# Gaps between the SBUF tiles that TensorE reads, so that they start at many different distances modulo 512 bytes

## The reference, cut to what matters

```python
# gated linear attention, per batch and head (D = 48)
for t in range(S):
    state = alpha[:, :, t, :, None] * state + einsum('bhd,bhe->bhde', k[:, :, t], v[:, :, t])
    y[:, :, t] = einsum('bhd,bhde->bhe', q[:, :, t], state)
# bilinear block: w1, w2 384x1024, w3 1024x1024, w_out 1024x384
h = ((x @ w1) * (x @ w2)) @ w3
x = h @ w_out
# four experts, all of them for every token: w1[e] 384x1024, w2[e] 1024x384
p = domain_probs / (domain_probs.sum(-1, keepdims=True) + 1e-09)
out += p[:, e:e + 1] * (np.maximum(x @ w1[e], 0.0) @ w2[e])
```

## Time and profile before

| | |
|---|---|
| median of 3 runs | 1226.57 us (1226.10 to 1228.07) |
| the profiled execution | 1225.81 us |
| its span, first to last instruction | 1224.1 us, so 1.7 us lie around it |
| TensorE (PE) busy | 1217.1 us, 99% |
| TensorE weight loads (PEld) busy | 1113.4 us, 91% |
| VectorE (DVE), ScalarE (ACT), GpSimd (POOL) busy | 453.1, 275.9, 168.1 us |
| mean granted TensorE clock | 1.000, the level of 2.4 GHz, throughout |

### The profile page before, as it was taken

One profiled execution on the slowest core, in us unless ns is written; L12 is line 12 of the kernel. 1 busy time (PEld: TensorE's weight loads), 2 busy tenths in 40 slices (PEclk: granted clock), 3 DMA queues, 4 the chain that ended last, 5 costly groups with the idle time before them and its releaser, 6 DMA issues.

```text
span 1224.1 us, 18775 instructions
## 1 busy us (share of the span) xinstructions
PE 1217.1 (99%) x7714; PEld 1113.4 (91%) x7714; DVE 453.1 (37%) x873; ACT 275.9 (23%) x515; POOL 168.1 (14%) x148
## 2 busy tenths in 40 slices
PE   9999999999999999999999999999999999999998
PEld 6699999999999999999999999999999999999998
DVE  4877775775751121222222222222222222222222
ACT  1433333333323311111111111111111111111111
POOL 1122222222222530000000000000000000000000
PEclk9999999999999999999999999999999999999999
DMA  9723643642613341011141111114001111222201
GB/s 286 220 71 84 180 118 73 183 119 70 169 47 139 123 182 38 19 47 52 52 155 52 52 51 51 52 52 154 18 35 51 52 52 52 78 77 77 78 6 46
DMA packets 84710, 107.49 MB, mean 88 GB/s; under 512 B 36384, under 2 KB 55072, under 8 KB 84128
## 3 DMA queue, kind: packets, MB, share of 16 engines
q1 hardware_dynamic: 84640, 106.50, 28.0%
HBM read 86.03 MB, written 18.09 MB: 85 GB/s over the span
## 4 chain that ended last, share of the span: by engine, by line
PE 96%; DVE 3%; ACT 0%; issue 0%; DMA 0%; DVEq 0%; SPq 0%
PE bank L1107 32%; PE bank L1216 25%; PE score_banks L1216 8%; PE bank L958 8%; PE bank L960 7%; PE bank L959 7%; PE bank L1150 2%; PE bank L997 2%; PE bank L1165 1%; PE score_banks L1018 1%; PE bank L1007 1%; PE score_banks L983 1%; DVE wb_lo L788 0%; DVE decay L726 0%; DVE suffix L704 0%
## 5 line engine op out<-in xcount | busy, mean ns | idle before, releaser
L782 DVE SCALAR_TENSOR_TENSOR h_lo<-bank,h_hi 128x512 fp32r<-128x512 f32 x192 | 132.8, 691 | 584.9 <-ACT h_hi L575 584.0
L575 ACT ACTIVATE h_hi<-bank 128x512 fp32r<-128x512 f32 x192 | 114.7, 597 | 661.7 <-PE bank L1107 661.7
L1107 PE MATMUL bank<-x_hi,we_lo 128*128 128x512 f32 x576 | 228.7, 397 | 0.0
L1107 PE MATMUL bank<-x_hi,we_hi 128*128 128x512 f32 x576 | 224.1, 389 | 0.0
L1107 PE MATMUL bank<-x_lo,we_hi 128*128 128x512 f32 x576 | 223.5, 388 | 0.0
L1216 PE MATMUL bank<-we_hi,h_hi 128*128 128x384 f32 x576 | 194.6, 338 | 0.0
L1216 PE MATMUL bank<-we_lo,h_hi 128*128 128x384 f32 x576 | 194.5, 338 | 0.0
L1216 PE MATMUL bank<-we_hi,h_lo 128*128 128x384 f32 x576 | 193.8, 336 | 0.0
L477 POOL TENSOR_TENSOR we_lo<-we_raw,we_hi (+1 forms) x48 | 60.9, 1291 | 527.3 <-ACT we_hi L536 527.3
L958 PE MATMUL bank<-x,wb_hi 128*128 128x384 f32 x384 | 128.7, 335 | 2.5 <-DVE g_sb L772 2.2
L1107 PEld LDWEIGHTS bank<-x_lo,we_hi 128*128 128x128 f32 x576 | 108.3, 188 | 22.7
(11 more groups left out here) (89 smaller groups left out, 1440.0 us busy)
## 6 DMA issues: line engine op xcount, KB each, us to landing
x_hi<-x_hi_spill SPq DMA_DIRECT2D x24, 768.0 KB, 4.9
x_lo<-x_lo_spill SPq DMA_DIRECT2D x24, 768.0 KB, 6.4
we_raw<-wset SPq DMA_DIRECT2D x4, 3072.0 KB, 10.2
inputs<-akq SPq DMA_DIRECT2D x24, 448.0 KB, 5.0
values<-v_rows SPq DMA_DIRECT2D x24, 256.0 KB, 3.5
inputs<-akq SPq DMA_DIRECT2D x24, 224.0 KB, 3.5
x_hi_spill<-x_hi_out SPq DMA_DIRECT2D x8, 576.0 KB, 4.2
x_lo_spill<-x_lo_out SPq DMA_DIRECT2D x8, 576.0 KB, 5.4
```

The costliest lines, as they stand in the source:

```text
L575: act.activation(h_hi[:, s % 2, :], bank[s % 2][:, :], ACT.Relu).then_inc(h_hi_ready, 1)
L782: dve.scalar_tensor_tensor(out=h_lo[:, s % 2, :], in0=bank[s % 2][:, :], scalar=0.0, in1=h_hi[:, s % 2, :], op0=ALU.max, op1=ALU.subtract) ...
L1107: mm = pe.matmul(bank[s % 2][:, :], (we_hi if term < 2 else we_lo)[e % 2][:, cols], (x1_lo if term == 1 else x1_hi)[u][:, k, :], start=(i ...
```

## The change

Nothing is computed otherwise. A helper `gap(words)` allocates a tile of so many float32 words that nobody uses, and such gaps are put between tiles; `h_hi` and `h_lo` are allocated after the small tiles instead of before them; `attention_rest`, an unused filler, is made smaller or larger so that the second set of expert weights still starts behind what it must not overwrite. In the built programs each engine has the same instructions in the same order with the same waits; only their line numbers and the addresses differ. Start of each tile modulo 512, in bytes, read from the two built programs:

The diff, whole but for context:

```diff
-ATTENTION_REST = ATTENTION_COLUMNS - 4 * KT * TILE2
+GAP_OF_WEIGHTS = 160
+ATTENTION_REST = ATTENTION_COLUMNS + GAP_OF_WEIGHTS - 4 * KT * TILE2 - 120 - 24 - 24 - 40
+        def gap(words, where=ctx):
+            gaps.append(words)
+            sb(f"gap{len(gaps)}", [P, words], F32, where)
+
+        gaps = []
-        h_hi = sb("h_hi", [P, 2, TILE2], F32R)
-        h_lo = sb("h_lo", [P, 2, TILE2], F32R)
         outside = sb("outside", [PD, BATCH * CHUNKS])
...
         alpha_range = sb("alpha_range", [PD, 2])
+        gap(80)
+        h_hi = sb("h_hi", [P, 2, TILE2], F32R)
+        gap(24)
+        h_lo = sb("h_lo", [P, 2, TILE2], F32R)
...
+        gap(GAP_OF_WEIGHTS, first)
         wb_hi = sb("wb_hi", [P, WSET], F32R, first)
+        gap(32, first)
...
         wb_lo = sb("wb_lo", [P, WSET], F32R, first)
+        gap(96, first)
         wp_hi = sb("wp_hi", [P, FT, DM], F32R, first)
+        gap(56, first)
         wp_lo = sb("wp_lo", [P, FT, DM], F32R, first)
-        x0 = [sb(f"x0_{t}", [P, CHUNKS1, KT + 1, 2, CHUNK], F32R, first) for t in range(TILES1)]
+        x0 = []
+        for t in range(TILES1):
+            gap((88, 56)[t], first)
+            x0.append(sb(f"x0_{t}", [P, CHUNKS1, KT + 1, 2, CHUNK], F32R, first))
...
+        gap(64, first)
         g_hi = sb("g_hi", [P, 2, TILE1], F32R, first)
+        gap(80, first)
         g_lo = sb("g_lo", [P, 2, TILE1], F32R, first)
...
+        gap(40, first)
...
         we_hi[0] = sb("we0_hi", [P, WSET], F32R, first)
+        gap(48, first)
...
         for slot in range(2):
+            gap((120, 24)[slot])
             x1_hi[slot] = sb(f"x1_{slot}_hi", [P, KT, TILE2], F32R)
+            gap((24, 40)[slot])
             x1_lo[slot] = sb(f"x1_{slot}_lo", [P, KT, TILE2], F32R)
         sb("attention_rest", [P, ATTENTION_REST])
+        gap(80)
         we_hi[1] = sb("we1_hi", [P, WSET], F32R)
+        gap(32)
```

## The result

Six runs of the changed kernel have a median of 1231.49 us (1230.92 to 1231.97); before stood at 1226.61 us (1225.90 to 1228.07, 6 runs). The ratio is 1.0039, 95% interval 1.0026 to 1.0052: the change makes the kernel 0.4% slower. The forecast was 1.7% slower, 1247.3 us.

The account below looks back on a forecast made before the run. The prediction took PE's gaps to bound the kernel: 8.1 us in stage 1 plus 12.6 us in stage 2, 20.7 us slower, made 1247.3 us. Its own range was 1235 to 1262, the 8-in-10 range 1206 to 1264.

Parts of the forecast that it names:

- What bounds the kernel: PE, busy 1217.1 of 1224.1 us and hardly waiting, so the sum of its gaps sets the end.
- the empty edits: Order and work unchanged on every engine, and the start's float32 matmuls at an unchanged distance: 0 each.
- the cover of the other engines: Work on g takes 2101 ns against PE's 3119 ns, leaving 1.0 us of cover a step: 0.
- the relative place of the operands: PE's gaps: some excess is contention of two operand reads, depending on how they lie in time and address.
- Stage 1: 1728 matmuls "up" and "down": gaps rise from 173.3 to 178.0 ns, 8.1 us slower.
- the unsettled gaps: Stage 1 gaps out of step after small attention matmuls, 178.0 ns each, taken as the cost at changing distances.
- Stage 2: 576 groups of four D and three U: 1408.6 ns against 1386.7 now, 12.6 us slower.
- D: Stage 2's "down" matmuls, 384 columns, four a group: 178.0 ns each forecast.
- U: Stage 2's "up" matmuls, 512 columns, three a group: 232.2 ns each forecast.
- the mixed case: Stage 2's steady groups before the change: excess of 15.2 ns a matmul, between pure streams at 13.3 and 18.9 ns.
- Rival A: Both stages: other distances keep reads apart, excess falls to 11 ns everywhere, 21.1 us faster, 1205.5 us; chance 0.28.
- Rival C: Only stage 1 loses, stage 2 being already out of step: 8.1 us slower, 1234.7 us; chance 0.15.

Follow-up runs that it names:

- e1: Small kernel of only float32r matmul streams, operand distances swept one at a time; excess over the columns 13.3 ns with both tiles moved together; no kernel time given.
- e8: Kernel before the change with every tile of both stages moved by the same 96 bytes modulo 512, all distances kept; 1226.64 us, ratio 0.9999.
- e5: The grid: small kernel running the D D U D U D U sequence at 64 pairs of distances, plus other widths and types; mean excess 116 ns a group of seven.
- e9: Small kernel alternating two float32r matmuls, distance off 0 within one or to the next one's stationary operand; excess 15.0 to 18.3 ns at the first distances.
- e4: Kernel before the change with x1 and the attention's tiles moved from 192 to 480, so every distance is 0; 1241.91 us, ratio 1.0117.
- e6: Kernel before the change with h at 96 and x1 at 0 modulo 512, the lowest of the 64 cases of e5; 1218.94 us, ratio 0.9937.
- e2: Changed kernel with h, we and x1 put back as before, so only stage 1's tiles stay moved; 1228.10 us, ratio 1.0015.
- e7: Kernel before the change with h and x1 both at 128 modulo 512, the worst case of e5; 1245.38 us, ratio 1.0123.

## Why the prediction was right and wrong

*What bounds the kernel, the empty edits, the cover of the other engines*: right. PE's gaps hold all 5.5 us; no wait appeared, `g` takes 2.10 us on the three engines as before.

*That the relative place of the operands counts*: right, shown by e1 (both moved: 13.3 ns) and e8 (0.9999), with two cases of e1 left open. It is not the only thing that counts: widths do too (e5, e9). One shape has gaps of 173.3 to 176.7 ns by addresses alone. The rule of the Trainium skill (page "TensorE: Matmul & The Clock Gate", section "Step-by-step: what each phase is for"), that loading the next weights takes no read bandwidth from the running matmul, says nothing of addresses, and these gaps do not follow from it. The prediction saw it contradicted by gaps of 173.3 and 178.0 ns, but both of those are at distance 0 and show only a stream before and after it settles. Nor is my reason shown, that the moving read runs side by side with the next matmul's load: e9 found an effect from both pairs, and a load of 32 columns costs as much as one of 128 at 384 columns and more at 512.

*Stage 1, (178.0 - 173.3) x 1728 = 8.1 us*: the mis-sized term. It measured 1.7 us. I took the 178.0 ns of the unsettled gaps for all distances that change from term to term, because "there is nothing that a repeating state can settle on". There is: settled patterns exist at every distance of e1, five of eight at the least excess of 13.3 ns and none over 16.7 (384 columns, steps of 32 bytes). The changed kernel, whose distances do change from term to term, settles as well: a stretch with `x0_1` repeats 172, 175 and 173 ns, 173.3 in the mean and no more than before, and one with `x0_0` has 175.6. The unsettled gaps are a way to a settled pattern, not a price list.

*Stage 2, 1408.6 - 1386.7 = 21.9 ns a group, 12.6 us*: it measured 6.4 ns and 3.7 us. D was the larger miss (175.1 against 178.0, four times 2.9 of the 15.5 ns that were too many) and is the same error; U came near (230.9 ns against 232.2). Beside it the sentence that the mixed case "lies between the two pure ones" was wrong in kind: with all distances 0 the sequence is worse than either pure stream (e4: 133 ns, 15 us slower).

What the grid puts in its place: a pair of distances drawn at random costs a group 113.5 (median) to 116 ns (mean) of excess, where before happened to have 106.7. Thus (113.5 to 116 - 106.7) x 576 = 3.9 to 5.4 us, and 3.7 us was lost. That the changed kernel behaves like such a draw is argued and not shown, for no run tried its own mix of distances in the small kernel. That before stood on a good cell could not be read from its own trace, which holds one case. So the direction was right in part by luck: the reason given for it, gaps that do not settle, is not what made the kernel slower. Rival A's figure of 11 ns everywhere is excluded by the 13.3 ns under which the mean of no settled pattern went; its direction, a faster kernel by other distances, is real, but only for the right pair (e6). Rival C came nearest (1234.7), with the wrong halves: it was stage 2 that lost more. One small slip changed nothing: a doubled GpSimd operation would show 0.005 us a step (2101 + 1023 - 3119 ns), not 0.02.

Still open: what in the chip has the period of 256 bytes, why the width of the neighbour matters, which reads meet, and what separates the two groups of times of e2 and e7.

## What to carry to other kernels

When PE never waits, look at the gaps from start to start in a steady stretch: where equal matmuls differ by some ns and repeat exactly, the relative addresses of the operands or the widths of the neighbours can be at work, and shifting tiles by 32 to 224 bytes was worth 0.6% or cost 1.2% here. Do not spread tiles at random and do not align them all: here that cost 5 and 15 us. Put the kernel's own sequence of matmuls into a small kernel, sweep the distances there in one run, and carry the best pair over; here that told the median time of two full kernels to 0.7 us, though one of the nine runs fell 12 us off.

## What the runs showed of the hardware that was not expected

- A settled stream of float32r matmuls has at least 13.3 ns of mean gap beyond its columns (120.0 ns at 256 columns, 173.3 at 384, 226.7 at 512), and still 13.3 with 32 or 64 stationary columns at 384. Other widths have more at the same distance 0: 16.0 ns at 448 columns, 31.7 at 192 (111.7 ns), 16 to 18 with 96 to 32 stationary columns at 512. bfloat16 has 2.5 ns, and so has each of the two instructions of a plain float32 matmul.
- The excess depends on the distance of the operands' addresses with a period of 256 bytes (e1, 16 distances at both widths), in float32r alone of the three types (bfloat16 was tried at four distances, float32 at three).
- It depends on the sequence as well: 384 and 512 columns in turn at distance 0 have 20.0 ns, 256 and 512 have 13.3 ns.
- A stream falls into an exactly repeating pattern of gaps, in stage 1 within six matmuls after a break, and one distance may have more than one such pattern (e1 at two distances, the runs of e7); that is not shown.
